# Attention scores two tiles ahead, and the copy of the transposed x on another engine

## What is computed

```python
for c in range(nc):                                   # 24 chunks of 32 positions
    q_c = q[:, :, c_start:c_end]
    k_full = concat([mem_k, k[:, :, l_start:r_end]])  # 8 + at most 56
    v_full = concat([mem_v, v[:, :, l_start:r_end]])
    scores = scale * (q_c @ k_full.T)
    scores = scores - max(scores, -1)
    a = exp(scores);  a = a / (sum(a, -1) + 1e-9)
    out[:, :, c_start:c_end] = a @ v_full
x = out.transpose(0, 2, 1, 3).reshape(3072, 512)
logits = x @ w_gate; noisy = logits + log1p(exp(x @ w_noise)) * noise
# the 2 best of 8 experts for each row, softmax over the two as weights
out[mask] += top2_w * (relu(x[mask] @ w1[e]) @ w2[e])   # first layer
# second layer: the best of 8 experts for each row, the same two products
```

## Time and profile before

| what | value |
|---|---|
| median of three runs | 1152.94 us (1152.82 to 1154.52) |
| profiled execution | 1152.72 us, of which the span of instructions is 1150.8 us |
| TensorE busy | 1096.4 us (95%) |
| VectorE busy | 642.8 us (56%) |
| ScalarE busy | 279.4 us (24%) |
| GpSimd busy | 320.8 us (28%) |
| mean granted TensorE clock | 0.976 of full |

### The profile page before, as it was taken

One profiled execution on the slowest core, in us unless ns is written; L12 is line 12 of the kernel. 1 busy time (PEld: TensorE's weight loads), 2 busy tenths in 40 slices (PEclk: granted clock), 3 DMA queues, 4 the chain that ended last, 5 costly groups with the idle time before them and its releaser, 6 DMA issues. The chain is left out here.

```text
span 1150.8 us, 29752 instructions
## 1 busy us (share of the span) xinstructions
PE 1096.4 (95%) x7973; PEld 884.7 (77%) x7974; DVE 642.8 (56%) x1360; ACT 279.4 (24%) x534; POOL 320.8 (28%) x474
## 2 busy tenths in 40 slices
PE   5989789999999999999999999999899999999997
PEld 4767666788888888888888888866578888888786
DVE  2767685655462553553645626415977425666863
ACT  3566321121212121212121121215212121212112
POOL 2004302323232332222322323220133223333332
PEclk8797999999999999999999999999999999999999
DMA  9999974877685775775867757449278646777963
GB/s 346 342 337 295 318 262 116 255 214 213 173 234 152 203 219 144 210 221 132 236 188 214 211 145 210 138 99 287 56 237 248 196 137 207 230 240 250 302 216 112
DMA packets 126990, 245.87 MB, mean 214 GB/s; under 512 B 17454, under 2 KB 70878, under 8 KB 126960
## 3 DMA queue, kind: packets, MB, share of 16 engines
q1 hardware_dynamic: 48608, 112.38, 29.6%
q10 hardware_dynamic: 61728, 90.25, 24.4%
q0 software_dynamic: 16624, 42.88, 16.8%
HBM read 169.51 MB, written 76.73 MB: 214 GB/s over the span
## 5 line engine op out<-in xcount | busy, mean ns | idle before, releaser
L1621 PE MATMUL moe_ps_y<-weights,moe_h_hi 128*128 (+1 forms) x624 | 254.0, 407 | 6.2 <-ACT moe_h_hi L1701 5.3
L1621 PE MATMUL moe_ps_h<-weights,moe_x_hi 128*128 (+1 forms) x640 | 251.4, 393 | 6.4 <-DVE moe_h_turned L1730 3.6
L1622 PE MATMUL moe_ps_h<-weights,moe_x_hi 128*128 (+1 forms) x640 | 249.4, 390 | 0.0
L1622 PE MATMUL moe_ps_y<-weights,moe_h_hi 128*128 (+1 forms) x624 | 246.5, 395 | 0.0
L1739 DVE SCALAR_TENSOR_TENSOR moe_h_lo<-moe_h_moved,moe_h_hi 128x256 fp32r<-128x256 f32 x312 | 111.6, 420 | 232.5 <-ACT moe_h_hi L1701 232.5
L1701 ACT ACTIVATE moe_h_hi<-moe_h_moved 128x1024 fp32r<-128x1024 f32 x78 | 82.7, 1061 | 382.4 <-PE moe_ps_y L1626 306.8
L1626 PE MATMUL moe_ps_h<-weights,moe_x_lo 128*128 (+1 forms) x640 | 171.4, 390 | 0.0
L147 DVE TENSOR_TENSOR weights<-stage,weights (+1 forms) x128 | 156.7, 1225 | 19.7 <-DVE weights L141 19.4
L1626 PE MATMUL moe_ps_y<-weights,moe_h_lo 128*128 (+1 forms) x624 | 154.2, 389 | 0.0
L1621 PEld LDWEIGHTS moe_ps_h<-weights,moe_x_hi 128*128 128x128 f32 x640 | 120.3, 188 | 38.1 <-issue 12.6
L1621 PEld LDWEIGHTS moe_ps_y<-weights,moe_h_hi 128*128 128x128 f32 x624 | 119.0, 191 | 31.6 <-issue 6.3
(11 more groups left out here) (269 smaller groups left out, 886.0 us busy)
## 6 DMA issues: line engine op xcount, KB each, us to landing
stage<-in_w SPq DMA_DIRECT2D x128, 512.0 KB
h_d<-moe_h_turned ACTq DMA_DIRECT2D x80, 512.0 KB
moe_h_moved<-h_d ACTq DMA_DIRECT2D x320, 128.0 KB
v_sb<-in_v SPq DMA_DIRECT2D x24, 520.0 KB, 5.3
k_sb<-in_k SPq DMA_DIRECT2D x24, 512.0 KB, 6.1
x_d<-zero SPq DMA_DIRECT2D x27, 260.0 KB, 7.1
q_sb<-in_q SPq DMA_DIRECT2D x24, 256.0 KB, 4.2
x_d<-x_sb ACTq DMA_DIRECT2D x24, 256.0 KB, 5.9
```

The source lines that it names most:

```text
L1621: pe.matmul(out, a_hi, b_hi, start=(i == 0), stop=False)
L1622: pe.matmul(out, a_hi, b_lo, start=False, stop=False)
```

## The change

Four things move.

1. The scores of a tile are issued one step earlier on TensorE: those of t+2 instead of t+1 stand behind the transposes of the exponentials of t. The scores of tile 2 come into the prologue. Loads of q and k are issued one tile earlier as well, so those of tile 3 now stand in front of the first four weight pieces on SyncE's queue.
2. The maxima and their negation run two tiles ahead on VectorE.
3. The copy of the transposed x goes from ScalarE to VectorE, behind the negation.
4. The store of x moves behind the exponentials of the next tile on ScalarE.

```diff
             load_v(1)
+            load_qk(2)
             for t in range(NT):
-                if t + 2 < NT:
-                    load_qk(t + 2)
+                if t + 3 < NT:
+                    load_qk(t + 3)
...
             p_transposes(0, 0)
+            scores(1, 0)
             values(0, 0).then_inc(sem("o_done"), 1)
             p_transposes(0, 1)
-            scores(1, 0)
+            scores(1, 1)
             x_transposes(0, 0)
...
                 p_transposes(r, 0)
-                scores(r, 1)
+                scores(r + 1, 0)
...
                 p_transposes(r, 1)
-                scores(r + 1, 0)
+                scores(r + 1, 1)
...
-            scores(r, 1)
             x_transposes(r - 1, 1)
...
                 copy_pT(t)
-                if t >= 1:
-                    copy_xT(t - 1)
-                    store_x(t - 1)
...
                 if t + 1 < NT:
                     probs(t + 1)
+                if t >= 1:
+                    store_x(t - 1)
...
+            def copy_xT(t):
+                dve.wait_ge(sem("xT_done"), t + 1)
+                if t >= 2:
+
+                    dve.wait_ge(sem("o_done"), t)
+                dve.tensor_copy(att.xT[t % 2][:, :, :], att.ps_x[:, :, :]).then_inc(sem("xT_ready"), 1)
+
...
             maxima(0)
             negate(0)
+            maxima(1)
+            negate(1)
             for t in range(NT):
                 if t == 9:
                     prepare_gate()
-                if t + 1 < NT:
-                    maxima(t + 1)
-                if t + 1 < NT:
-                    negate(t + 1)
+                if t + 2 < NT:
+                    maxima(t + 2)
+                    negate(t + 2)
+                if t >= 1:
+                    copy_xT(t - 1)
...
+            copy_xT(NT - 1)
             copy_logits(NT - 1)
```

More of the change, by code:

```diff
@@ L912, in copy_pT @@
                 act.copy(att.pT[t % 2][:, :, :], att.ps_p[:, :, :]).then_inc(sem("pT_ready"), 1)
[L914 to L919, removed]
             def store_x(t):
@@ L949, in _ @@
                     probs(t + 1)
+                if t >= 1:
+                    store_x(t - 1)
                 if t in LN:
                     noise_ln(LN[t])
-            copy_xT(NT - 1)
             store_x(NT - 1)
```

## The result

The changed kernel takes 1155.33 us (median of 20 runs, 1150.32 to 1163.75) against 1151.90 for the kernel before (20 runs, 1148.79 to 1156.22). The ratio is 1.0032, with a 95% interval of 1.0016 to 1.0047: slower by 3.4 us. The time lies inside the forecast's range, but the direction was wrong: 1.0 us less was forecast. That it is still inside is luck: the upper end of the range came from rival C with a copy of 0.93 us, and the copy takes 0.69.

What follows compares the result with a forecast made beforehand. At full clock a chain through exponentials, transposes, scores and maxima paces the attention; at half clock TensorE does. 2.5 us gained less 1.5 lost gives 1.0 less, from 1152.72 to 1151.7 us, range 1147.5 to 1156.3.

Steps and rivals of the forecast that it cites:

- rival C: VectorE becomes the slower bound: copy costs 0.93 us, 2.9 us more, plus 0.8 of half clock; 1155.4 us, chance 0.16.
- The copy's length: Copy of xT out of PSUM on VectorE: taken as 0.69 us, against about 0.34 by the SBUF copy's row.
- The step that failed: Attention tiles at full clock: VectorE sets the pace in 12; each 0.34 less is 4.1 us less, 0.24 more 2.9 more.
- Rival B: Attention: denser TensorE keeps the clock up, 13.6 us of half clock go, 3.1 us less; 1148.6 us, chance 0.21.
- Tiles 21 to 23: End of the attention: these tiles have 3.8 us of slack before the expert layer's first transposes.
- Tiles 10 to 20: Attention tiles with other VectorE work: mean 4.67 us against 4.98 over 8.2 full-clock tiles, a gain of 2.5 us.
- Tile 13: Attention tile where VectorE was already late: stays as long as before.
- tiles 11, 12 and 18: Attention tiles that were to become shorter; table loads had delayed the exponentials of 11 and 18.
- Tiles 5 to 7: Attention tiles with weight pieces: 4.72 us each against 4.34, a loss of 1.1 us.
- The start: First tiles, scores and loads of q and k earlier: counted 0, with ends -1.1 and +2.3 us.
- The end: Second slots lead to the expert layer's first transposes, so tiles up to 20 move the end one for one.

Runs made afterwards that it cites:

- k3: Kernel before, cut off behind the attention stage, with only the copy of xT on VectorE and the store of x behind the exponentials: 147.20 us.
- g1: Kernel before, cut off behind the attention stage, otherwise unaltered: 144.26 us.
- k2: Changed kernel, cut off behind the attention stage, with only the start put back to the order of before; copy stays on VectorE: 148.95 us.
- g3: Changed kernel, cut off behind the attention stage, with the start of before and copy and store of x back on ScalarE: 145.93 us.
- g2: Changed kernel, cut off behind the attention stage, otherwise unaltered: 151.69 us.
- k1: Changed kernel, cut off behind the attention stage, with only the copy of xT and the store of x back on ScalarE: 145.88 us.
- f3: Full changed kernel with one added matmul of zeros a tile between values and gate: 1156.03 us, 1.0032 to the kernel before.
- e3: Full changed kernel with only the copy of xT and the store of x back on ScalarE: 1156.10 us, 1.0041 to the kernel before.
- i1: The same kernel as e3, measured again: 1154.00 us, 1.0038 to the kernel before.
- e1: Full changed kernel with only the start (early scores, loads of tile 3) put back to the order of before: 1155.78 us, 1.0037 to the kernel before.
- e2: Full changed kernel with the first four weight pieces loaded one a step, steps 0 to 3: 1156.57 us, 1.0046 to the kernel before.
- h1: Full changed kernel with the start of before and copy and store on ScalarE, leaving the order two ahead: 1152.53 us, 1.0006 to the kernel before.
- a0: Changed kernel unaltered, measured again for a second profile: 1156.12 us, 1.0031 to the kernel before.
- f2: Full changed kernel with one added matmul of zeros a tile behind the gate: 1156.19 us, 1.0031 to the kernel before.
- g4: Changed kernel, cut off behind the attention stage, with the first four weight pieces loaded one a step: 151.40 us.

## Why the prediction was wrong

- **The copy's length** was right (690 ns against 0.69), and so was what took its place: the wait of the gate for `xT` in tiles at full clock, none left for `pr`. The rule on PSUM reads in the Trainium skill (VectorE: DVE Perf Modes, "Why PSUM operands drop a tier") agrees: 690 ns, and not the 0.34 us of the row of the SBUF copy.
- **The step that failed is the one that priced the copy on VectorE by VectorE's length alone** ("In 12 tiles VectorE sets the pace at the full clock"), with the clock's stretches carried over from before. The forecast left the time at half clock as it was, a term of 0; rival C had 0.8 us for it. In its place the runs showed 14.9 us more at half clock in the full kernel (64.6 against 49.7). At 0.184 that is 2.7 of the 4.4 us between the forecast and the measured time; the rest is not put down to anything. In the stage by itself the copy on VectorE goes with 18 us more at half clock alone (k3 against g1), 12 with the order two ahead (k2 against g3) and 28 within the change (g2 against k1), and it costs 3 to 6 us there. By what path it does so is not shown. In the first profile the waits of the gate for the late copy, up to 1.62 us in one piece, are followed by half clock; in the second most of the half clock does not stand behind such waits.
- **Rival B had the sign wrong.** TensorE did get denser from 62 to 86 us (18.90 to 19.97 busy), but the time at half clock rose from 49.7 to 64.6 us.
- **Tiles 21 to 23** were counted as having slack. They hold the one-hot rows on VectorE. With the copy there the profiles have them at 16.1 to 17.7 us (15.6 once, in f3), against 13.6 to 15.8 in the kernels with the copy on ScalarE and the start of before. The longest wait for `xT` stands in them. The copy is not alone in this: with the start of the changed kernel they took 16.2 to 17.8 us also with the copy on ScalarE (k1, e3, i1).
- **Tiles 10 to 20** gained 1.5 us in the first profile (57.84 to 56.3 from `den` 9 to `den` 20), where 2.5 were forecast. In the second profile they lost 1.4 (59.2), and with the copy on VectorE and the order two ahead e1, e2 and k2 took 57.7, g2 60.8. So the gain of 2.5 us cannot be counted on. Tile 13 was about as long as before (4.48 against 4.68), as said. Of tiles 11, 12 and 18, which were to be shorter, only tile 11 was (3.92 against 5.39); 12 took 4.60 against 4.46 and 18, with a stretch at half clock in it, 6.40 against 5.68. In the cut kernels the order alone gained nothing either (58.7 against 57.8): with the copy on ScalarE the wait for the exponentials stays.
- **Tiles 5 to 7** were to take 4.72 each; they took 14.15/3 = 4.72 in the first profile. The 1.1 us of loss were right.
- **The start** was counted 0 with an end of +2.3. The first profile had 2.5 us of loss there, but k1 against g3 shows that in the cut stage it costs nothing by itself. In e1 `den` of tile 4 is still 1.9 us late, so e1 does not test it.
- **The end** followed the second slots, as argued (1.48 us of the 2.20), with 0.7 us more from the tiles behind them.

Left open: why the start of the changed kernel, with the copy on ScalarE, costs nothing in the cut stage (k1) and 0.4% in the full kernel (e3 and i1). The difference to h1 in time at half clock is 7 to 12 us (54.8 and 59.6 against 48.0), which at 0.184 is 1 to 2 us of some 4 by the ratios.

## What to carry to other kernels

When work is moved to an engine that is idle on average, look for the tiles in which that engine has its bursts: if TensorE waits for the moved result there, the move can cost more than the length of the wait, since the time at half clock may change with it. Price such a move with a term for the clock, bounded by the time of a tile at either clock. Where runs spread by more than the effect, cut the stage out and time it alone; here that took the spread from some 12 us to some 5 (over fewer runs) and told parts apart that the full kernels had not. It also doubled the effect, for a reason not found, so what it gives is the order of the parts and not their price in the whole.

## What the runs showed of the hardware

- About the same idle time on TensorE in the cut stage (30.9 and 28.5 us) went with 31 and with 62 us at half clock. What differs is where the idle time stands: 9.4 us for the exponentials in 16 pieces before; 4.8 us for the copy in 6 and 2.6 for x in 5 after. That the waits cause the falls of the clock was read from the order of events in the first profile and from the copy's edits, and is not shown: a0 had 61 us at half clock up to 144 us with 2.0 us of such waits, and f2 and f3 put matmuls beside these waits and took 10 of the 15 us away without a gain in time.
- Half clock lasted with TensorE fully busy, in a0 for 13.7 us at a time:

```profile
88.50:102.20 13.70, 13.70 (x350) 11.20 (x333) 11.21 (x41) 6.52 (x29) 10.12 (x14) 0.52 0.78 274
```

- The stop of TensorE in the first pass through the loop (2.63 us before, 4.34 after) ends in both kernels 1.3 to 1.4 us behind the end of a fetch of instructions of 16 KB (started at 24.2 and 19.9 us, 0.9 to 1.0 us long), while loads move 370 to 380 GB/s. That the fetch queues behind the loads was not tested apart from e2 and g4, which did not settle it.
